# Prologue of a fused attention, MoE and MLP kernel: the second half batch's values in their own place, the first one's logarithm chain and inverse ahead of the second's, three banks for its decay

## The reference, cut to what matters

```python
mag = np.sqrt(a_re * a_re + a_im * a_im)
scale = np.minimum(mag, 0.999) / (mag + 1e-06)
a_re_n, a_im_n = (a_re * scale, a_im * scale)
for t in range(S):                       # S = 768, for B = 4, H = 8, D = 48
    ar, ai = (a_re_n[:, :, t, :, None], a_im_n[:, :, t, :, None])
    new_re = ar * S_re - ai * S_im
    new_im = ar * S_im + ai * S_re
    kv = np.einsum('bhd,bhe->bhde', k[:, :, t], v[:, :, t])
    S_re, S_im = (new_re + kv, new_im)
    y[:, :, t] = np.einsum('bhd,bhde->bhe', q[:, :, t], S_re)
# x = y as 3072 rows of 384; then, per row, the expert of the largest logit:
out[mask] = gate_w[mask, None] * (np.maximum(xe @ w1[e], 0.0) @ w2[e])
# and on its output
h = (x @ w1) * (x @ w2) @ w3
return h @ w_out
```

## Time and profile before

| | |
|---|---|
| median of 3 runs | 1012.51 us |
| the profiled execution | 1015.03 us |
| its span | 1013.3 us, 17941 instructions |
| PE, PEld busy | 924.8 us (91%), 818.8 us (81%) |
| DVE, ACT, POOL busy | 439.8, 412.1, 394.7 us (43%, 41%, 39%) |
| mean granted TensorE clock | 0.98 of full speed |

### The profile page before, as it was taken

One profiled execution on the slowest core, in us unless ns is written; L12 is line 12 of the kernel. 1 busy time (PEld: TensorE's weight loads), 2 busy tenths in 40 slices (PEclk: granted clock), 3 DMA queues, 4 the chain that ended last, 5 costly groups with the idle time before them and its releaser, 6 DMA issues.

```text
span 1013.3 us, 17941 instructions
## 1 busy us (share of the span) xinstructions
PE 924.8 (91%) x6799; PEld 818.8 (81%) x6799; DVE 439.8 (43%) x703; ACT 412.1 (41%) x620; POOL 394.7 (39%) x230
## 2 busy tenths in 40 slices
PE   1678999889889699989999999998999999999996
PEld 1568888778878466979999999997898989898986
DVE  2559889979967360252222222222313131313130
ACT  4768798688654232232322322321222222222221
POOL 6336476676745342573373657610010101010101
PEclk9779999999999999999999999999999999999999
DMA  7714434534365147541532553411010101000000
GB/s 200 137 33 95 87 72 79 126 79 81 78 186 189 41 176 234 172 136 61 164 112 101 165 172 103 166 40 48 1 63 1 63 1 63 1 32 1 32 1 32
DMA packets 160151, 91.81 MB, mean 91 GB/s; under 512 B 128576, under 2 KB 152896, under 8 KB 160064
## 3 DMA queue, kind: packets, MB, share of 16 engines
q1 hardware_dynamic: 147344, 67.81, 25.1%
q10 hardware_dynamic: 9648, 13.30, 4.2%
q0 software_dynamic: 3072, 9.49, 2.4%
HBM read 71.77 MB, written 18.81 MB: 89 GB/s over the span
## 4 chain that ended last, share of the span: by engine, by line
PE 71%; DVE 15%; POOL 5%; issue 5%; ACT 2%; another core or an unknown queue 1%; DMA 0%; SPq 0%; ACTq 0%; DVEq 0%; POOLq 0%
PE psum L1840 19%; PE psum L1799 13%; PE psum L1777 12%; PE psum L1852 10%; PE psum L401 6%; PE psum L1686 4%; PE psum L1623 2%; DVE arena L1182 2%; DVE arena L1114 2%; DVE arena L1133 1%; PE psum L1649 1%; POOL x_by_expert L690 1%; DVE arena L1121 1%; POOL arena L671 1%; POOL arena L659 1%
## 5 line engine op out<-in xcount | busy, mean ns | idle before, releaser
L1840 PE MATMUL psum<-x2t,ring 128*128 128x512 f32 x864 | 197.1, 389 | 0.0
L1840 PEld LDWEIGHTS psum<-x2t,ring 128*128 128x128 f32 x864 | 162.1, 188 | 33.5
L401 PE MATMUL psum<-arena 128*128 128x128 f32 x925 | 130.3, 283 | 38.3 <-DVE arena L1114 21.9
L401 PEld LDWEIGHTS psum<-arena 128*128 128x128 f32 x925 | 110.2, 146 | 53.7 <-issue 42.8
L784 POOL DMA_INDIRECT out_dram<-arena x24 | 23.1, 963 | 320.9 <-ACT arena L1093 317.4
L1777 PE MATMUL psum<-ring,f_xt 128*128 x558 | 137.2, 400 | 4.4 <-DVE f_xt L1474 4.4
L1799 PE MATMUL psum<-ring,f_ht 128*128 x744 | 138.7, 341 | 2.0 <-DVE f_ht L1480 2.0
L1799 PEld LDWEIGHTS psum<-ring,f_ht 128*128 128x128 f32 x744 | 129.7, 190 | 2.4 <-issue 2.3
L1777 PEld LDWEIGHTS psum<-ring,f_xt 128*128 128x128 f32 x558 | 103.7, 190 | 26.0 <-issue 4.9
L1515 DVE TENSOR_TENSOR ab_f<-psum,a_sb 128x512 f32<-128x512 f32 x48 | 33.2, 692 | 204.6 <-ACT a_sb L1083 204.6
L1852 PE MATMUL psum<-wfold_half,ab 128*128 128x384 f32 x576 | 102.8, 336 | 0.0
(11 more groups left out here) (178 smaller groups left out, 1371.1 us busy)
## 6 DMA issues: line engine op xcount, KB each, us to landing
stage<-in_moe_w_dram SPq DMA_DIRECT2D x16, 1536.0 KB, 7.3
y_dense<-arena ACTq DMA_DIRECT2D x31, 194.0 KB, 2.7
arena<-x_by_expert ACTq DMA_DIRECT2D x28, 194.0 KB, 2.4
arena<-y_dense SPq DMA_DIRECT2D x24, 194.0 KB, 3.6
arena<-in_a_re_dram SPq DMA_DIRECT2D x24, 192.0 KB
arena<-in_a_im_dram SPq DMA_DIRECT2D x24, 192.0 KB
arena<-in_q_dram SPq DMA_DIRECT2D x24, 192.0 KB, 2.7
arena<-in_k_dram SPq DMA_DIRECT2D x24, 192.0 KB, 3.4
```

The costliest lines, as they stand in the source:

```text
L401: return nc.tensor.transpose(psum[:, bank, c0:c0 + P], src, ident)
L1840: last = mm(psum[:, bank + j % 2, :], m_half[m][x][:, kc, j * P:(j + 1) * P], x2t[y][:, kc, :], start=(kc == 0 and x + y == 0), stop=(kc = ...
```

## The change

Unit 1's raw values get buffers of their own (`a_second`), in the place of unit 1's later scan and root buffers, and its s3 and s4 too. Both units' values are loaded first, ahead of the blocks of m3 and m_out. Steps -4 to -1 are replaced by a list per engine. In it unit 0's three chunks use three banks each for decay and phases, with no wait between them; `clip`(0) comes ahead of `ratio`(0), and its minimum waits only for the first half of `damp`; unit 0's logarithm (`seed_inv_log`, `seed_inv`), `inverse`, `sines` and `cosines` move ahead of the second unit's chain or of the fold; unit 1's squares are made by VectorE instead of ScalarE; `ratio`(1) and the rest of unit 1's `clip` fall into step 0, and unit 1's chunks are prepared in steps 0 (one) and 1 (two) instead of -1, 0 and 1. From step 2 on the lists are those of before.

```diff
+        a_second = [cols(second_at + x * ND, ND) for x in range(2)]
+        s3_second, s4_second = [cols(second_at + (2 + x) * ND, ND) for x in range(2)]
...
+        def prepared(k):
+            return {0: [K], 1: [K + 1, K + 2]}.get(k, [k + AHEAD] if k + AHEAD < K * U else [])
+        def decay_bank(n, i):
+            return A2_BANK if n else (A2_BANK, Q_BANK, K_BANK)[i]
+        def phase_bank(n, i):
+            return PH_BANK if n else (PH_BANK, A_BANK, A_BANK + 1)[i]
@@ SP
             load_a(0)
+            load_a(1)
             load_m3(0, m3_early)
             sp.dma_start(mo_early, ...)
             load_m3(1, m3_early)
-            load_a(1)
@@ GpSimd
+                if k == 0:
+                    root_prod(0, 0)
+                    ratio_seed(1)
+                    root_prod(0, 1)
+                    root_prod(0, 2)
...
                     turn_q(n, i)
+                if k == 0:
+                    sum_angles(1)
...
             add_squares(0)
             ratio_seed(0)
             route_consts()
-            for k in range(-4, K * U + 1):
+            sum_angles(0)
+            add_squares(1)
+            for k in range(0, K * U + 1):
@@ ScalarE, whole_turns
+                if n == 1:
+                    act.wait_ge(r_checked, 2)
@@ ScalarE, step: after angle(p)
+                for a in prepared(k)[:-1]:
+                    whole_turns(*divmod(a, K))
@@ ScalarE
+            logs()
             act.wait_ge(consts, 9)
-            logs()
             squares(0)
             seed(0)
             damp(0)
             trig()
             angle(0)
-            for k in range(-4, K * U + 1):
+            ratio_check(0)
+            whole_turns(0, 0)
+            logs()
+            seed_inv_log(0)
+            whole_turns(0, 1)
+            whole_turns(0, 2)
+            seed_inv(0)
+            seed(1)
+            damp(1)
+            fold_rows(0, fold_out)
+            trig()
+            turn_abs(0)
+            sines(0)
+            cosines(0)
+            angle(1)
+            fold_rows(1, fold_out)
+            for k in range(0, K * U + 1):
@@ VectorE, clip
-                dve.wait_ge(damp_done, 2 * m + 2)
+                dve.wait_ge(damp_done, 2 * m + 1)
                 V.tensor_scalar(s1, s1, MAG2_MAX, None, ALU.min).then_inc(clip_done, 1)
                 dve.wait_ge(clip_done, m + 1)
+                dve.wait_ge(damp_done, 2 * m + 2)
@@ VectorE
+            def squares_second():
+                dve.wait_ge(a_loaded[1], 16 * 2 * K)
+                dve.wait_ge(a2_done, 1)
+                V.tensor_tensor(s1, a_second[0], a_second[0], ALU.mult).then_inc(sq_done, 1)
+                V.tensor_tensor(s2, a_second[1], a_second[1], ALU.mult).then_inc(sq_done, 1)
@@ VectorE, scan
+                if n == 1 and i == 0:
+                    dve.wait_ge(r0_done, 2)
@@ VectorE, step
+                if k == 0:
+                    weigh_inputs(0, 0)
+                    clip(1)
+                    ratio(1)
+                    scan(1, 0)
+                    turn_k(0, 0)
+                    clear_y()
...
+                    for a in prepared(k):
+                        scan(*divmod(a, K))
+                        if a != prepared(k)[-1]:
+                            turn(*divmod(a, K))
@@ VectorE
             unit_check(0)
+            clip(0)
             ratio(0)
-            clip(0)
-            for k in range(-4, K * U + 1):
+            for i in range(K):
+                scan(0, i)
+            squares_second()
+            for i in range(K):
+                turn(0, i)
+            ends(0)
+            fold_cols(0, m3t_early)
+            fold_cols(1, m3t_early)
+            inverse(0)
+            unit_check(1)
+            for k in range(0, K * U + 1):
@@ TensorE, inputs_t
+                if k0 == 0:
+                    pe.wait_ge(scan_done, K)
@@ TensorE, fold_t
+                    else:
+                        pe.wait_ge(turn_done, half + 2)
@@ TensorE, step
-                if 0 <= a < K * U:
+                for a in prepared(k):
                     decay_cols(*divmod(a, K))
+                    if a != prepared(k)[-1]:
+                        phases(*divmod(a, K))
@@ TensorE
-            for k in range(-4, K * U + 1):
+            for i in range(K):
+                decay_cols(0, i)
+            for i in range(K):
+                phases(0, i)
+            fold_t(0, m3_early)
+            fold_t(1, m3_early)
+            inputs_t(0, 0)
+            fold(0, m3t_early, mo_early)
+            fold(1, m3t_early, mo_early)
+            for k in range(0, K * U + 1):
```

More of the change, by code:

```diff
@@ L440, in load_a @@
             def load_a(m):
[L441 to L444, removed]
+                if m >= 2:
+                    done = 1 if m == 2 else m
+                    sp.wait_ge(r0_done, done)
+                    sp.wait_ge(unit_e, done)
+                for dst, src in zip(raw_a(m), (a_re, a_im)):
                     for i in range(K):
-                        sp.dma_start(dense(dst)[:, i], unit_of(src, m)[:, i]).then_inc(a_loaded, 16)
+                        sp.dma_start(dense(dst)[:, i], unit_of(src, m)[:, i]).then_inc(a_loaded[m % 2], 16)
             def load_qk(k):
@@ L926, in step @@
                 n, i = divmod(k, K)
-                m, p, a = n + 1, n + 2, k + AHEAD
-                if 0 < a <= K * U:
-                    whole_turns(*divmod(a - 1, K))
+                m, p = n + 1, n + 2
+                if k and prepared(k - 1):
+                    whole_turns(*divmod(prepared(k - 1)[-1], K))
                 if k >= 2:
@@ L937, in step @@
                         logs()
-                    if 0 < p < U:
+                    if p < U:
                         squares(p)
-                if i == 1 and 0 < p < U:
+                if i == 1 and p < U:
                     seed(p)
@@ L966, in step @@
                         exp_logits((k - PICKED - 1) // C)
-                    if 0 <= m < U:
+                    if m < U:
                         seed_inv_log(m)
-                if i == 2 and 0 <= m < U:
+                if i == 2 and m < U:
                     turn_abs(m)
-                if k == -1:
-                    fold_rows(1, fold_out)
+            logs()
             act.wait_ge(consts, 9)
-            logs()
             squares(0)
@@ L1298, in step @@
                 n, i = divmod(k, K)
[L1299 to L1303, removed]
+                m, p = n + 1, n + 2
+                if k and prepared(k - 1):
+                    a = prepared(k - 1)[-1]
+                    turn(*divmod(a, K))
+                    if a % K == K - 1:
+                        ends(a // K)
                 if i == 2 and k >= PICKED + 2 and (k - PICKED - 2) % C == 0:
                     weigh((k - PICKED - 2) // C)
-                if i == 2 and 0 < p < U:
+                if i == 2 and p < U:
                     ratio(p)
-                if k == -1:
-                    fold_cols(0, m3t_early)
-                    fold_cols(1, m3t_early)
                 if 1 <= k <= K * U:
@@ L1319, in step @@
                     place((k - PICKED - 1) // C)
-                if 0 <= a < K * U:
-                    scan(*divmod(a, K))
+                if k:
+                    for a in prepared(k):
+                        scan(*divmod(a, K))
+                        if a != prepared(k)[-1]:
+                            turn(*divmod(a, K))
                 if i == 0 and k >= PICKED and (k - PICKED) % C == 0:
                     pick((k - PICKED) // C)
-                if i == 1 and 0 < p < U:
+                if i == 1 and p < U:
                     unit_check(p)
                     clip(p)
-                if i == 2 and 0 <= m < U:
+                if i == 2 and m < U:
                     inverse(m)
-                if k == 0:
-                    clear_y()
                 if k == K * U - 2:
@@ L1691, in step @@
                 n, i = divmod(k, K)
-                a = k + AHEAD
                 if k >= 2:
@@ L1715, in step @@
                         key_rows(k - 1)
-                if 0 <= a < K * U:
+                for a in prepared(k)[-1:]:
                     phases(*divmod(a, K))
```

77 lines of the change are left out of this document (40 added, 37 removed).

## The result

The changed kernel takes 1001.41 us (median of 4 runs, 999.18 to 1001.67) against 1013.16 us: ratio 0.9886, 95% interval 0.9862 to 0.9911, 11.75 us between the medians. Two further comparisons of the same two kernels, on chips 1 and 6, gave 0.9849 (0.9823 to 0.9875) and 0.9845 (0.9822 to 0.9868), 15.5 and 14.4 us between medians. The time lies in the range and within 1 us of the forecast; over the three comparisons the gain is rather 14 than 12 us.

What follows compares the result with a forecast made beforehand. The prologue's chain of waits was taken to bind, with the inverse behind the fold delaying the first mask. Mask 14.3 us earlier, less 2.1 of moved work, gives 12.2; 1012.51 - 12.2 = 1000.3, said as 1000.5 us, range 994 to 1007.

Steps and rivals of the forecast that it cites:

- Step 1: Transfers: unit 1's values queue behind unit 0's; cost taken as nothing, bounds nothing to 4.88 us.
- Step 2: `clip`(0) ahead of `ratio`(0), with VectorE and GpSimd blocking each other: a2 1.5 us earlier, the angle 1.9 us later.
- Step 3: Three banks for unit 0's chunks: third `phases` ends at 30.4 us, bounds 28.8 and 32.1.
- Steps 4 and 5: ScalarE's and VectorE's lists: unit 1's squares hidden, `inverse`(0) ends at 38.1 us instead of 62.75.
- Step 6: VectorE and GpSimd in step 0: instructions reading two SBUF tensors alternate; `ratio`(1) ends at 49.1 us, lower bound 44.7.
- Step 7: The fold: `fold`(0) takes 6.67 or 5.19 us, sine and cosine don't bind; cost nothing.
- Step 8: Up to the mask: `turn`(1,0) waits for ScalarE; `mask`(0) at 58.6 instead of 72.91, less 2.1 us moved behind it.
- B: Rival: TensorE stays at 1.2 GHz in the prologue; gain 9.9 us, time 1002.6 us; chance 0.12.
- C: Rival: ScalarE's lag in steps 1 to 3 gives back 4 to 7 us; 1005 to 1008 us; chance 0.20.
- D: Rival: ScalarE isn't stopped, the scores bind the mask at about 54.5; gain 16 to 17 us, 996; chance 0.08.
- A: The main case, all steps as forecast: 999 to 1002 us, gain 13.5 with the third `phases` at 28.8; chance 0.50.
- F: Rival: slower, one more VectorE instruction per unit falls behind a GpSimd one; 1016.5 us, 1032 if both; chance 0.05.

Runs made afterwards that it cites:

- e9: The changed kernel with unit 0's inverse made to wait for both of the fold's matmul groups; 1011.3 us, ratio 0.9984 to the kernel before.
- e1: The changed kernel with unit 1's values loaded behind the blocks of m3 and m_out, as before; 1001.1 us, ratio 0.9870 to the kernel before.
- e6: The changed kernel with unit 1's values loaded only once unit 0's are read, and behind m3; 1000.9 us, ratio 0.9880 to the kernel before.
- e2: The changed kernel with `ratio`(0) ahead of `clip`(0) again; 1001.2 us, ratio 0.9858 to the kernel before.
- e5: The changed kernel with unit 1's squares back on ScalarE, ahead of unit 0's logarithm; 1002.4 us, ratio 0.9904 to the kernel before.
- e3: The changed kernel with unit 0's `seed_inv` behind unit 1's seed and damp on ScalarE; 1005.1 us, ratio 0.9908 to the kernel before.
- e4: The changed kernel with one bank each for unit 0's decay and phases, and the waits of before; 1006.5 us, ratio 0.9947 to the kernel before.

## Why the prediction was right, step by step

**The mechanism** held: the inverse ahead of the fold, carried through a first mask that starts much earlier, less 2.05 us of scan and turn moved behind it. By the profiled pair: 17.9 us at the mask and 15.9 at a2 of unit 2, a subtraction as the prediction made it; by the means of two and three profiles 16.1 and 14.0. e9 shows that, with the rest in place, the gain stands or falls with the early inverse. Carrying the lead on unchanged was right too.

**Step 1** took the transfers at nothing. e1 and e6 show 0.2 to 0.5 us in favour of the change; the bounds given excluded a gain, which was wrong.

**Step 2** was right to 0.2 us: from the first squares' start to the end of `ratio`(0) it is 20.2 - 8.3 = 11.9 us, in the sum 21.5 - 9.4 = 12.1, and the blocking is the one it named. The Trainium skill's rule ("SBUF — State Buffer", "Who interferes with whom") agrees with these rows. What step 2 held against the swap was not so: e2 shows that the earlier a2 is worth more than the delayed angle.

**Step 3** was the term most in error. The third `phases` was put at 30.4 us, with a bound of 28.8; by the profile it ended at 27.85. Of these 2.6 us 1.1 are the earlier start. Another 0.5 are the transposes: the sum takes 3 x 1.08, but the twelve in a row took 2.79. The rest, 0.9, is the cadence, which became fast at 24.9 us, 5.8 us after TensorE's first transpose, in the second `phases` and not in the third:

```profile
24.22 0.63 PE L1644 MATMUL psum<-arena 128*128 128x128 f32 x2
24.64 0.52 PE L1646 MATMUL psum<-arena 128*128 128x128 f32 x2
25.00 0.39 PE L1644 MATMUL psum<-arena 128*128 128x128 f32 x2
```

These are pairs of matmuls in TensorE's timeline of the kernel after; a pair starts every 0.43 us up to there and every 0.22 us from there on. The place is not fixed: in the two other profiles of the changed kernel it lies at about 23.3 and 24.0 us. And the window of 22 to 24 us gives a granted clock of 1.00 in spite of the slow pairs, so in this stretch the spacing of the matmuls tells the cadence and that column doesn't.

**Steps 4 and 5.** `turn`(0,2) ended at 29.2 (31.7), the inverse at 35.5 (38.1), `unit_check`(1) at 36.8 (39.5): the same 2.5 to 2.7 us throughout, so the durations were right. The squares were hidden, as taken (e5).

**Step 6** held: `ratio`(1) 9.0 us after `unit_check`(1), 9.6 in the sum, by the alternation drawn up there. Its reason is put too simply: not all of these instructions read two SBUF tensors. The minimum (L1164) reads one and was held up all the same; the weighing (L1226) reads one beside PSUM and wasn't. **Step 7** held: the fold binds nothing, and its first half took 5.3 us, not 6.7. **Step 8** named the new wait: VectorE stood idle 5.58 us for `whole_turns`(1,0). From the end of `ratio`(1) to the mask it was 9.2 us, 9.5 in the sum. The scores began at 49.0 us instead of 52 to 54 and took 2.1 instead of 3.81, which changed nothing, as they didn't bind. The mask came at 55.05 instead of 58.6.

**The rivals.** B: no; in all three profiles of the changed kernel the third `phases` ran at the fast cadence. C (part given back): no; from a2 of unit 2 to the flag `bad` it is 241.5 and 242.7 us before, 241.5, 241.9 and 242.6 after. In some of the experiments, with the same list from step 2 on, it is up to 244.5 (e6), so 2 to 3 us can be lost there in an execution. D: its start of the mask (54.5) is nearer to the measured one than A's (58.6), but not by its cause, since ScalarE was stopped twice (1.5 and 1.8 us) and the exclusion didn't fall otherwise; and the gain of 14.0 is nearer A's 13.5 than D's 16. F: a2's instruction takes 3.68 us in all six later units, `ratio` 1.34, as before.

**The size** fell 2 us short of the mean gain (12.2 against 14), by two errors against each other. The mask was put 3.6 us too late: 1.1 by the start, 1.4 by step 3, 0.1 by steps 4 and 5, 0.6 by step 6 and 0.3 by step 8. And the one profile before that served as the base had its mask 1.5 us later than the mean of two. That the forecast time fell within 1 us of the first measured median is in part luck.

What stays open: why unit 0's values land up to 0.45 us apart from one execution to the next in the same kernel; what sets the place of the slow clock; the worth of the separate buffers alone; and that of `ratio`(1) and `clip`(1) in step 0 and of the earlier minimum in `clip`, which applies to all units. No run undid these.

## What to carry to other kernels

When an engine that works through a list has a short, early-ready instruction behind a long foreign stage, move it ahead, and check what else must be out of its way: here the early inverse needs the three banks and, for its last 3 to 4 us, the early logarithm chain (e3). Taking away the banks (e4) takes away two thirds of the gain, taking away the inverse's place (e9) nearly all of it; no run has one of them alone. Subtract from the lead at the first full engine what was moved behind it; that difference, not the lead, arrives at the end. And profile the base twice before sizing a few microseconds: its prologue alone varied by 3 us.

## What the runs showed of the hardware

VectorE and GpSimd took strict turns in the kernel after from 37.9 to 46.9 us: three of VectorE's instructions and three of GpSimd's each waited for one of the other's, and each of VectorE's took 2.3 to 2.5 us instead of 0.75 to 1.36. Two of the three (L1169, L1183) read two SBUF tensors, the third (L1164) one; an instruction with one input in SBUF and one in PSUM (L1226) took its usual 0.69 us beside GpSimd. In the profile such a wait stands inside the instruction, as busy time: a2's takes 3.68 us in the later units against 1.36 alone.

The granted clock around the first scores was 0.50 in a different stretch in each execution of one kernel (66 to 74 us in the first profile before, 64 to 66 in the second; in the kernel after 56 to 58 in the first profile, 48 to 50 in the third). So the same 32 matmuls of the scores took 3.81 us or 2.08 us before, 2.65 or 2.06 after.
